# Another order of the 18 slots of a turn in a fused convolution and two-layer MLP kernel

## The reference

```python
# x: (4, 4096, 192), weight: (8, 7); w1_in, w2_in: (192, 2048); w1_out, w2_out: (2048, 192); all float32
w = exp(weight - max(weight)); w = w / (sum(w) + 1e-9)          # per head, 8 heads of 24 columns
x1[b, s, :] = sum over k in 0..6 of w[head, k] * x[b, s - 6 + k, :]   # zero ahead of the start
h  = x1 @ w1_in;  x2  = (h * cos(h)) @ w1_out                   # layer one ("A")
h  = max(x2 @ w2_in, 0);  out = (h * h) @ w2_out                # layer two ("B")
```

## Time and profile before

| | |
|---|---|
| median of 3 runs | 2569.09 us (2557.86 to 2569.69) |
| the profiled execution | 2572.67 us, its span 2570.9 us |
| TensorE matmul busy | 2391.5 us, 93% |
| VectorE busy | 1902.8 us, 74% |
| ScalarE busy | 1776.4 us, 69% |
| GpSimd busy | 24.5 us, 1% |
| mean granted clock | 0.968 |
| DMA | 33.05 MB, mean 13 GB/s |

### The profile page before, as it was taken

How to read it: one execution, slowest core, us unless ns; L and a number is a source line. 1 busy time by engine, 2 the same in 40 slices (tenths; PEclk the granted TensorE clock), 3 DMA queues, 4 the chain that set the end, 5 groups by cost and what they waited for, 6 DMA issues and landing times.

```text
span 2570.9 us, 49058 instructions
## 1 busy us (share of the span) xinstructions
PE 2391.5 (93%) x20352; PEld 2086.2 (81%) x20352; DVE 1902.8 (74%) x2125; ACT 1776.4 (69%) x1872; POOL 24.5 (1%) x11
## 2 busy tenths in 40 slices
PE   4699999999999999999999999999999999999998
PEld 3588888888888888888888888888888888888886
DVE  7777777778777778777778777778777778777761
ACT  4477677676677776677676677676677676777674
POOL 1200000000000000000000000000000000000000
PEclk9799999999999999999999999999999999999999
DMA  3100000000000000000000000000000000000000
GB/s 104 31 7 14 13 7 12 9 9 12 12 6 12 6 12 12 12 6 12 6 12 12 12 6 12 6 12 12 12 6 12 6 12 12 11 8 6 6 7 13
DMA packets 39308, 33.05 MB, mean 13 GB/s; under 512 B 1516, under 2 KB 38508, under 8 KB 39020
## 3 DMA queue, kind: packets, MB, share of 16 engines
q1 hardware_dynamic: 39100, 32.58, 4.3%
q10 hardware_dynamic: 176, 0.00, 0.0%
HBM read 19.99 MB, written 12.58 MB: 13 GB/s over the span
## 4 chain that ended last, share of the span: by engine, by line
PE 59%; DVE 21%; ACT 11%; issue 8%; DMA 0%; ACTq 0%; DVEq 0%; SPq 0%
PE h L349 8%; PE h L355 7%; PE h L353 7%; PE h L351 7%; DVE w L705 6%; DVE w L703 3%; PE y_A L388 3%; PE y_A L390 3%; ACT w L604 3%; PE y_A L392 3%; PE y_A L394 3%; PE y_A L396 3%; PE y_B L394 3%; ACT g L594 3%; PE y_B L388 3%
## 5 line engine op out<-in xcount | busy, mean ns | idle before, releaser
L717 DVE TENSOR_TENSOR g_lo<-g,g_hi 128x1024 fp32r<-128x1024 f32 x512 | 629.6, 1230 | 348.2 <-ACT g_hi L615 346.3
L615 ACT ACTIVATE g_hi<-g 128x1024 fp32r<-128x1024 f32 x512 | 537.5, 1050 | 161.2 <-DVE g L712 160.0
L604 ACT ACTIVATE w<-w,quarter 128x1024 f32<-128x1024 f32 x256 | 295.1, 1153 | 298.8 <-DVE w L705 298.8
L349 PE MATMUL h<-x_side_A,up_side_A 64*128 64x512 f32 x1024 | 410.6, 403 | 95.6 <-DVE x_side_A L752 86.9
L349 PE MATMUL h<-x_side_B,up_side_B 64*128 64x512 f32 x1024 | 409.0, 401 | 67.4 <-ACT g L596 47.2
L388 PE MATMUL y_A<-g_hi,dn_lo_A 64*128 64x512 f32 x1024 | 425.7, 416 | 5.1 <-DVE g_lo L717 4.9
L390 PE MATMUL y_A<-g_hi,dn_hi_A 64*128 64x512 f32 x1024 | 416.5, 407 | 0.0
L594 ACT ACTIVATE g<-h 128x1024 f32<-128x1024 f32 x256 | 261.6, 1022 | 223.9 <-PE h L355 223.9
L396 PE MATMUL y_A<-g_lo,dn_side_A 64*128 64x512 f32 x1024 | 414.4, 405 | 0.0
L394 PE MATMUL y_A<-g_hi,dn_side_A 64*128 64x512 f32 x1024 | 413.2, 403 | 0.0
L392 PE MATMUL y_A<-g_lo,dn_hi_A 64*128 64x512 f32 x1024 | 413.2, 403 | 0.0
(11 more groups left out here) (96 smaller groups left out, 6336.5 us busy)
## 6 DMA issues: line engine op xcount, KB each, us to landing
rows_in<-x SPq DMA_DIRECT2D x32, 384.0 KB, 3.2
out<-late SPq DMA_DIRECT2D x32, 384.0 KB, 2.6
late<-w_out SPq DMA_DIRECT2D x2, 1536.0 KB, 10.1
g<-w_in SPq DMA_DIRECT2D x1, 1024.0 KB, 5.2
g<-w_in SPq DMA_DIRECT2D x2, 512.0 KB, 8.0
late<-w_in SPq DMA_DIRECT2D x2, 512.0 KB, 4.5
late<-w_in SPq DMA_DIRECT2D x4, 256.0 KB, 5.6
taps<-weight ACTq DMA_DIRECT2D x4, 0.7 KB
```

Source lines behind the costliest of these rows:

```text
L349: mm = pe.matmul(dst, up_side[kind][rows, f], xin_side[kind][rows, :], start=rows is top, stop=z)
L604: act.activation(v, v, ACT.Sin, bias=quarter[:, 0:1], scale=-TURN).then_inc(cosine, 1)
L615: act.activation(g_hi[:, r, :, :], g[:, r, :, :], ACT.Copy).then_inc(hi_made[kind], 1)
L717: dve.tensor_tensor(g_lo[:, r, :, :], g[:, r, :, :], g_hi[:, r, :, :].bitcast(F32), ALU.subtract).then_inc(lo_made[kind], 1)
```

## The change

The list `SLOTS`, the slots of the taps and of the split, and the slots in which y_A and y_B are read are different. `FIRST_SLOTS` is not. VectorE's `split_layer1` was in slot SPLIT_SLOT + 1 = 16 and is in SPLIT_SLOT = 16 now, so only ScalarE's part of the split moves, from 15 to 16.

```diff
-SLOTS = [("A", 0), ("A", 1), ("A", 2), ("B", 0), ("X", 0), ("B", 1), ("A", 3), ("B", 2), ("A", 4),
-         ("B", 3), ("A", 5), ("Y", 0), ("A", 6), ("B", 4), ("A", 7), ("B", 5), ("B", 6), ("B", 7)]
+SLOTS = [("A", 0), ("A", 1), ("B", 0), ("A", 2), ("B", 1), ("A", 3), ("X", 0), ("B", 2), ("A", 4),
+         ("B", 3), ("B", 4), ("A", 5), ("A", 6), ("A", 7), ("B", 5), ("B", 6), ("Y", 0), ("B", 7)]
...
-TAP_SLOTS = (5, 5, 7, 9, 11, 13, 15)
+TAP_SLOTS = (6, 7, 9, 9, 10, 14, 15)
 FIRST_TAP_SLOTS = (11, 11, 12, 13, 14, 15, 15)
-SPLIT_SLOT = 15
+SPLIT_SLOT = 16
...
# ScalarE: the read of y_A, then of y_B
-                    if s == 1 and turn.runs("A", 1):
+                    if s == 0 and turn.runs("A", 1):
...
-                    if s == 4 and turn.runs("Y"):
+                    if s == 3 and turn.runs("Y"):
...
# VectorE: split_layer2, the sum for y_B, split_layer1
-                    if s == 1 and turn.runs("A", 1):
+                    if s == 0 and turn.runs("A", 1):
                         split_layer2(turn)
...
-                    if s == 4 and turn.runs("Y"):
+                    if s == 3 and turn.runs("Y"):
...
-                    if turn.runs("X") and s == SPLIT_SLOT + 1:
+                    if turn.runs("X") and s == SPLIT_SLOT:
```

## The result

The changed kernel takes 2377.32 us (median of 4 runs, 2376.41 to 2377.91) against 2568.01 before in the same series (2557.86 to 2569.69): ratio 0.9265, 95% interval 0.9240 to 0.9289. The profiled execution has a span of 2375.7 us and a mean clock of 0.990. The forecast was 2388, range 2362 to 2448.

What follows compares the result with a forecast made beforehand. TensorE bounds the loop; a turn falls from 77.37 to 71.2 us. 29 turns give -178.9, with -4.4, -1.8, 0 and +3 that is -182: 2390.6 from the profiled 2572.7, on the median's level 2387, stated as 2388, range 2362 to 2448.

Steps and rivals of the forecast that it cites:

- The bound and the three waits: TensorE bounds the loop turn; waits for x_side_A, h and g_lo cost 4.55 us, leaving 71.0 without them.
- A0's chain, 7.4 against 7.15: Slot 0: ScalarE and VectorE need 7.4 us until x1_made, TensorE's slots 16 and 17 cover 7.15; 0.2 us wait stays.
- the first rival: A0's chain 1.2 us late, a slow piece following in two of three turns: 2451 us; chance 0.22.
- B0 and B1: Waits for g_lo (0.55 us) and the read of h (1.41) go, with 0.8 and 1.0 us in hand.
- The margins in slots 3 to 15: Moved X, y_B copies and taps cost 0; least margins 0.7 us at slot 12, 1.2 at 7, 1.3 at 8.
- the fourth rival: Three A pairs in slots 11 to 13 run slower than TensorE's pace: 2653 us at 7.3 each; chance 0.03.
- the second: Rival: VectorE, not TensorE, sets the pace and the waits reappear elsewhere, no net change, 2569 us; chance 0.03.
- The clock: With no wait near 1.8 us left, no half-speed piece in the loop turns; granted clock 1.00.
- The third rival: Transposes alone lower the clock, a slow piece behind X and Y each turn: 96 us more, 2484; chance 0.05.
- The start: Turn 0: split behind the late weights' copies lets them and GpSimd's subtraction start 1.8 us sooner: -1.8, between -2 and 0.
- The end: Last two turns, layer two alone: 58.5 work, 2 waits, 8 last copies and store, 5 half speed: 74 us, +3 (-2 to +12).
- The sum: Whole kernel: 29 turns -178.9, then -4.4, -1.8, 0 and +3, together -182 us.

Runs made afterwards that it cites:

- VectorE's split first: Kernel before with VectorE's split_layer1 moved ahead of slot 16's low part: 2501.12 us, ratio 0.9755.
- Y's read taken out of the chain: Changed kernel with ScalarE's split ahead of the read of Y in slot 16: 2367.37 us, ratio 0.9227.
- The undone read: Changed kernel with the read of y_A and its split put back from slot 0 to slot 1 on ScalarE and VectorE: 2617.32 us.
- the tail alone: Kernel before with only Y moved to slot 16, y_A read in slot 0, split in slot 16, taps fitted: 2393.3 us, ratio 0.9329.
- the front alone: Changed kernel's slots 0 to 9 and y_A, y_B reads, with the old list from slot 10, split in 15/16, other taps: 2505.31 us, ratio 0.9763.
- old tap rhythm: Changed kernel with taps in slots (6, 6, 7, 9, 11, 13, 15): 2417.19 us, ratio 0.9423.
- two activations more: Changed kernel with two unused 64x512 copies added inside ScalarE's split: 2418.78 us, ratio 0.9413.
- four activations more: Changed kernel with four unused 64x512 copies added inside ScalarE's split: 2504.75 us, ratio 0.9749.

## Why the prediction was right, step by step

- **The bound and the three waits.** Right. With TensorE's work untouched, a turn lost 6.36 us, for 6.17 forecast. The turn without waits was put at 71.0 from the earlier trace rows and is 70.68: the small sums for a matmul's modelled end and for the longer slot behind a wait (3 x 0.16 and 3 x 0.1) would have had to be 0.12 larger for each wait, 0.38 and not 0.26. VectorE's split first fits the same: 70.68 + 1.07 + 0.55 + 1.43 + 3 x 0.38 = 74.9, its turn without a slow piece.
- **A0's chain, 7.4 against 7.15.** Right in mechanism and nearly in size: 0.33 us remain, 0.2 forecast; with Y's read taken out of the chain it is gone. The wait with its upper end of 1.2 (the first rival) did not come.
- **B0 and B1.** Right: no wait, and B0's margin was 0.7 for 0.8. The undone read (5.86 us idle) shows the chain as it was worked out. What I had not seen is how the parts hang together: by the tail alone B1's wait falls to 0.5, and the front alone brings a new one of 0.69.
- **The margins in slots 3 to 15.** No wait showed. That they are tight there was right (the old tap rhythm costs 1.34 us a turn), how tight was overstated: 2.4 forecast, as ScalarE's 0.80 us ahead of B6's read were not counted. With it the fourth rival loses much of its ground, and VectorE as the bound (the second) is out, as TensorE's matmuls have no hole.
- **The clock.** Right that it would be 1.00. The third rival fell: each turn has its 28 transposes, and there is no piece at half speed in 29 turns. The rule that it was taken from (the Trainium skill, TensorE: Matmul & The Clock Gate, Part 4: PE-mode transpose) may hold for a stretch of transposes alone, which no run here shows; woven with other matmuls, the transposes did nothing to the granted clock here.
- **The start.** Forecast -1.8, found -3.2: A0 of turn 1 starts at 100.56 instead of 103.74. The right sign, but not by the sum of the prediction, which shifted everything by the 1.8 of the three split activations. The split had also waited 4.3 us for the taps ahead of it, so that without it GpSimd's subtraction starts 6.1 us sooner, at 88.46 instead of 94.60, and stands beside other work (timeline of GpSimd and VectorE, turn 0, to be held against the earlier trace rows):

```profile
88.46 4.55 POOL L818 TENSOR_TENSOR dn_lo_B<-late,dn_hi_B 128x2048 fp32r<-128x2048 f32 x1 [16.62 <-ACT dn_hi_B L567]
```

```profile
88.54 5.02 DVE L744 SCALAR_TENSOR_TENSOR conv_side<-xt_side,taps,conv_side 64x512 f32<-64x512 f32 x1
93.59 2.71 DVE L742 SCALAR_TENSOR_TENSOR conv<-xt,taps,conv 128x512 f32<-128x512 f32 x1
```

Two taps (5.02 and 2.71 us, 0.75 elsewhere) take the blow, and the low part and the split are spared. The first ends 0.6 us behind GpSimd's instruction (88.46 + 4.55). That again fits a port pair taken in turns (the Trainium skill, SBUF — State Buffer, SBUF: two separate sides). Turn 1, put at 0, gave back 1.2 of the 3.2: from A0 of turn 1 to A0 of turn 2 it is 77.4 us and not 76.2.

- **The end.** Wrong, the one term with the wrong sign: +3 forecast, -3.0 found. Two terms were mis-sized by nearly 3 us each. The windows view cuts the stretch into its part at full clock, the half-speed piece, the rest of the matmuls and what lies behind the last one:

```profile
2307.30:2343.50 36.20, 33.45 (x221) 26.54 (x219) 10.40 (x12) 20.81 (x22) 0.00 (x0) 1.00 0.00 1
2343.50:2346.90 3.40, 3.40 (x16) 2.75 (x15) 0.35 (x1) 0.00 (x0) 0.00 (x0) 0.50 0.00 0
2346.90:2371.80 24.90, 22.89 (x161) 18.12 (x159) 4.36 (x4) 11.02 (x12) 0.00 (x0) 0.98 0.05 16
2371.80:2375.70 3.90, 0.00 (x0) 0.00 (x0) 0.00 (x0) 0.81 (x1) 0.00 (x0) 0.50 0.31 101
```

Half speed cost some 2.2 us (1.7 in the piece, 0.5 in the next line) and not 5; the low clock of the last 3.9 us, where no matmul runs, cost nothing, and so the mean of 0.94 overstates it. The same chain at full clock is then 66.2 us and not 69: 3.9 us, not 8, lie behind the last matmul. In the kernel before, a piece of 10.2 us had cost some 5. TensorE's waits of over 0.15 us in this stretch add up to 3.9 us, 8.1 before, so the new order's longer cover between a pair's up and its down took half of them; that the clock held up because of it is likely and not shown by a run of its own.
- **The sum.** -182 forecast, -195.2 in the spans: 5.5 of the rest is the turn (29 x 0.19), 6 the end, the others the start, turn 1 (+1.2) and turn 31.

What the clock cost, read over all kernels: idle time of a wait, and how many of 29 turns had a half-speed piece behind it.

| kernel, wait | idle us | turns with a piece |
|---|---|---|
| VectorE's split first, A0 | 1.07 | 0 |
| old tap rhythm, A0 | 1.15 | 0 |
| two activations more, A0 | 1.21 | 0 |
| before, B1 | 1.41 | 14 |
| VectorE's split first, B1 | 1.43 | 3 |
| before, A0 | 1.81 | 19 |
| front alone, A0 | 1.81 | 22 |
| four activations more, A0 | 2.52 | 29 |
| y_A read in slot 1, B0 | 5.86 | 29, of 6.8 us in 25 of them, begun within the wait |

Between 1.2 and 2.5 us the price of a wait at these places goes from itself to itself and 1.6 us. Why the same wait at B1 brought 14 pieces in one kernel and 3 in another stays open; in the kernel before, an earlier wait of 1.81 stands in the same turn, and one of 1.07 in the other. The table holds for these full turns alone. With layer two alone, where the stream is thinner, waits of the small size did not leave the clock up: in the kernel before, a wait of 1.13 us ended at 2512.1, and 2.0 us later a long piece began.

```profile
2514.10:2524.30 10.20, 9.09 (x39) 6.42 (x37) 2.85 (x3) 4.38 (x5) 0.00 (x0) 0.50 0.00 0
```

## What to carry to other kernels

In an order written by hand, count for each wait of the bounding engine what stands ahead of it in the queues of the others, in the order in which they run it; here one read ahead of a split was worth 10 us of 2377, and one low part ahead of two subtractions 65 us of 2566. Moving the output's transposes (Y) to slot 16, by which A7's down and so y_A are done a slot sooner, with the taps, the split and the read of y_A fitted to it, gave nine tenths of the gain. The read of y_A has to move with it, or the change is a loss. And a long wait can cost more than itself: cutting one from 1.81 to 1.07 us gave 2.33 us a turn, three times what it measured, since 30 of 33 half-speed pieces went with it. Waits of up to 1.21 us had no such piece behind them in the full turns, but one of 1.13 us did where layer two runs alone.

## What the runs showed of the hardware

TensorE's granted clock fell to half behind single pauses of 1.4 to 2.5 us in a stream that is otherwise full, in some turns or in all, for 3.4 us each time (at 2.5 us these began up to 0.3 us ahead of the next matmul), and never behind the transposes woven into it (28 a turn, 29 turns at 1.00). Behind pauses of 1.07 to 1.21 us it did not fall in such a stream; in the thinner one at the end of the kernel before, it did within 2.0 us of a pause of 1.13. In pauses of 5.9 us it fell while TensorE still stood still, up to 4.0 us ahead of the next matmul, and stayed at half for 6.8 us in 25 of 29 turns, of which 3.6 us on the mean met matmuls. Beside a GpSimd instruction of 4.55 us, a VectorE instruction that takes 0.75 us elsewhere took 5.02 us.
